# Second layer of a fused attention and two-layer network: gate and value as seven block products of 462 tokens in place of eight products of 512

## What is computed

```python
# attention: p_packed = sm_attn(p, k, v); out = sm_attn(q, p_packed, p_packed)
# x: (4608, 512)
h = x @ w_in                                   # 512 -> 2048
g = np.maximum(h, 0.0) + alpha * np.minimum(h, 0.0)
y = g @ w_out                                  # 2048 -> 512
# second layer, the one that the change rewrites
gate = y @ w_gate                              # 512 -> 1536
silu = gate * (1.0 / (1.0 + np.exp(-gate)))
val = y @ w_val                                # 512 -> 1536
out = silu * val @ w_out2                      # 1536 -> 512
```

## Time and profile before

| | |
|---|---|
| median of 3 runs | 1685.91 us (1685.32 to 1686.03) |
| the profiled execution, whole | 1685.89 us |
| its span, first to last instruction | 1683.7 us |
| TensorE busy | 1662.8 us (99%) |
| VectorE busy | 811.6 us (48%) |
| ScalarE busy | 568.6 us (34%) |
| granted TensorE clock, mean | 1.000 |

### The profile page before, as it was taken

How to read it: one execution, slowest core, us unless ns; L and a number is a source line. 1 busy time by engine, 2 the same in 40 slices (tenths; PEclk the granted TensorE clock), 3 DMA queues, 4 the chain that set the end, 5 groups by cost and what they waited for, 6 DMA issues and landing times.

```text
span 1683.7 us, 23290 instructions
## 1 busy us (share of the span) xinstructions
PE 1662.8 (99%) x9454; PEld 1480.7 (88%) x9454; DVE 811.6 (48%) x1524; ACT 568.6 (34%) x1229; POOL 19.1 (1%) x33
## 2 busy tenths in 40 slices
PE   9999999999999999999999999999999999999998
PEld 6899989999999999999888888888888888888887
DVE  4777678776976768656423232222323232232322
ACT  4565567555855566445201010100101010010100
POOL 0000000000000000000000000000000000000000
PEclk9999999999999999999999999999999999999999
DMA  7343223221322222124201010000101000010000
GB/s 254 102 121 114 85 73 95 77 82 49 111 63 78 70 65 68 40 76 135 84 1 51 0 51 0 25 26 0 51 1 51 0 26 25 1 50 0 26 0 26
DMA packets 51098, 94.83 MB, mean 56 GB/s; under 512 B 4896, under 2 KB 13104, under 8 KB 50992
## 3 DMA queue, kind: packets, MB, share of 16 engines
q1 hardware_dynamic: 48656, 83.90, 15.8%
q0 software_dynamic: 2336, 9.45, 1.6%
HBM read 74.46 MB, written 18.87 MB: 55 GB/s over the span
## 4 chain that ended last, share of the span: by engine, by line
PE 93%; DVE 4%; ACT 2%; issue 1%; DVEq 0%; ACTq 0%
PE acc L737 12%; PE h L531 9%; PE h L529 9%; PE h L530 9%; PE side L529 8%; PE side L530 8%; PE side L531 8%; PE acc L529 7%; PE acc L531 7%; PE acc L530 7%; PE acc L741 6%; DVE piece L1086 1%; ACT floats L823 1%; DVE floats L1254 1%; PE side L619 0%
## 5 line engine op out<-in xcount | busy, mean ns | idle before, releaser
L737 PE MATMUL acc<-g,w 128*128 128x288 f32 x1792 | 272.2, 294 | 0.0
L737 PEld LDWEIGHTS acc<-g,w 128*128 128x128 f32 x1792 | 249.0, 188 | 0.0
L1279 DVE TENSOR_TENSOR floats<-side,floats 128x512 f32<-128x512 f32 x54 | 37.4, 692 | 323.5 <-PE side L531 323.5
L823 ACT ACTIVATE g<-floats 128x288 fp32r<-128x288 f32 x256 | 113.8, 444 | 215.4 <-PE acc L741 104.9
L1279 DVE TENSOR_TENSOR floats<-h,floats 128x512 f32<-128x512 f32 x54 | 37.3, 691 | 266.2 <-PE h L531 266.2
L1254 DVE SCALAR_TENSOR_TENSOR floats<-floats,h 128x288 f32<-128x288 f32 x256 | 130.6, 510 | 61.1 <-ACT floats L983 59.5
L1086 DVE TENSOR_TENSOR g<-floats,g 128x288 fp32r<-128x288 f32 x256 | 115.4, 451 | 91.4 <-ACT g L823 89.5
L1086 DVE TENSOR_TENSOR piece<-floats,piece 128x512 fp32r<-128x512 f32 (+1 forms) x191 | 131.6, 707 | 57.9 <-ACT piece L823 55.8
L529 PE MATMUL h<-attn,mixed 128*128 128x288 f32 x512 | 156.9, 307 | 1.7 <-DVE attn L1086 1.7
L1012 ACT ACTIVATE floats<-side 128x512 f32<-128x512 f32 x54 | 32.3, 599 | 372.3 <-PE side L531 372.3
L741 PE MATMUL acc<-g,w 128*128 128x288 f32 x896 | 156.1, 296 | 0.0
(11 more groups left out here) (168 smaller groups left out, 3351.5 us busy)
## 6 DMA issues: line engine op xcount, KB each, us to landing
floats<-w_in SPq DMA_DIRECT2D x64, 256.0 KB, 3.0
y_scratch<-floats POOLq DMA_DIRECT2D x16, 576.0 KB, 3.6
floats<-y_scratch SPq DMA_DIRECT2D x9, 1024.0 KB, 5.0
out<-floats SPq DMA_DIRECT2D x36, 256.0 KB, 2.5
floats<-kT SPq DMA_DIRECT2D x28, 288.0 KB, 2.9
floats<-qT SPq DMA_DIRECT2D x28, 288.0 KB, 2.8
floats<-vS SPq DMA_DIRECT2D x28, 256.0 KB, 2.7
early<-w_in SPq DMA_DIRECT2D x16, 256.0 KB, 8.1
```

The costliest lines, as they stand in the source:

```text
L737: pe.matmul(acc[:, m, 0:CH], w2[:, j, x, m * P:(m + 1) * P], g[:, s % 2, 0, :], start=False, stop=False)
L823: return nc.scalar.activation(dst, src, ACT.Copy, **kw)
L1279: nc.vector.tensor_tensor(u_float(j), val_bank[j % 2], sg[:, j % 2, :], ALU.mult).then_inc(u_ready, 1)
```

## The change

Only the second layer's arithmetic is new, but it needs things prepared in the first layer.

**Block products.** Tokens now go in 5 runs (`HALF`: four of 2 x 462 and one of 2 x 456). Take the gate and value weights of one tile j as a 2 x 2 matrix of blocks: a11, a12 are the two feature halves of gate, a21, a22 those of value. Take the 512 features by 924 tokens of y as blocks B11, B12 (first feature half, first and second token half), B21, B22. The four results (gate and value of both token halves) come from seven products (`TERMS`) in place of eight: a11 B11, s2 T2, s1 T1, a22 T4, s3 T3, a12 B21, s4 B22, where s1 = a21 + a22, s2 = s1 - a11, s3 = a11 - a21, s4 = a12 - s2 and T1 = B12 - B11, T2 = B22 - T1, T3 = B22 - B12, T4 = B21 - T2. A product has 2 x 3 matmuls of 462 columns. A *set* n is the seven terms of one tile j in one run; there are 60. Four terms open a PSUM bank, three add to one after ScalarE or VectorE has read it.

**Work on VectorE and ScalarE.** A set's four results are put together from the banks: `copy_first`, `silu_1`, `silu_2` on ScalarE, `set_start` and `set_rest` on VectorE. Down for the first token half runs inside the sets, down for the second half (from a kept float tile `u2`) in a second loop of 12 tiles after them; there the next run's blocks are made and split as well (`T_STEPS`, 22 steps).

**Weights.** SBUF does not hold all seven split weight blocks of 12 tiles. So gate and value pieces and the sums s1 to s4 are made and split inside the first layer, at twelve places (`KEEP_AT`), and stored to a DRAM scratch `wS` by 48 DMAs from GpSimd; the second layer reads each set's 1.8 MB (four DMAs of SyncE, `load_weights`) into one of two places in turn, 60 times. Only the down weights stay.

```diff
+HALF = [462, 462, 462, 462, 456]
+TERMS = [("B11", 0), ("T2", 1), ("T1", 2), ("T4", 3), ("T3", 1), ("B21", 0), ("B22", 2)]
+KEEP_AT = [62, 73, 79, 97, 117, 141, 162, 181, 202, 208, 214, 220]
...
-WEIGHT_SLOT = [LAST + 6, LAST + 7] + [LAST + 8 + n for n in range(8)] + [LAST + NT1 + 1 + n for n in range(15)]
...
+MID[LAST + 1] += [("yload",), ("wload",)]
+for _n in range(len(T_STEPS)):
+    BACK[LAST + 4 + _n // 2].append(("tstep", _n))
...
+            def load_weights(n):
+                if n == 0:
...
+                elif n >= 2:
+                    once.wait_ge(term_done, 7 * (n - 2) + 7)
+                for i in range(4):
...
+                    sp.dma_start(ring(n, i).bitcast(F32), src).then_inc(weights_landed[n % 2], 16)
...
+            def term(n, i):
...
+                if i == 0:
+                    once.wait_ge(weights_landed[n % 2], 64 * (n // 2 + 1))
...
+                elif i == 6:
+                    once.wait_ge(value2_ready, n + 1)
+                w, x = term_weights(n, i), block_of(name)
+                for k in range(2):
+                    mm = product(bank_groups[r % 2][bank][:, 0:h], hl(lambda a: w[:, a, k * P:(k + 1) * P]),
+                                 hl(lambda a: x[:, a, k, 0:h]), i < 4 and k == 0, k == 1, skip_group_check=True)
...
-            for c in range(NC2):
+            for r in range(RUNS):
                 for j in range(NT2):
...
+                    n = NT2 * r + j
+                    for i in range(2 if n == 0 else 0, 6):
+                        term(n, i)
+                    if j:
+                        down_tile(2 * NT2 * r + j - 1)
+                    term(n, 6)
+                for d in range(NT2 - 1, 2 * NT2):
+                    down_tile(2 * NT2 * r + d)
...
+            def sums(j):
...
+                nc.vector.tensor_tensor(s1_, a21, a22, ALU.add).then_inc(sums_step, 1)
+                nc.vector.tensor_tensor(s3_, a11, a21, ALU.subtract).then_inc(sums_step, 1)
...
+            def set_rest(n):
+                r, j = divmod(n, NT2)
+                h, bank = HALF[r], bank_groups[r % 2]
+                once.wait_ge(term_done, 7 * n + 5)
+                nc.vector.tensor_tensor(first_three[:, 0:h], bank[1][:, 0:h], first_term[:, 0:h], ALU.add
+                                        ).then_inc(three_ready, 1)
+                once.wait_ge(three_ready, n + 1)
+                nc.vector.tensor_tensor(value2[:, 0:h], bank[2][:, 0:h], first_three[:, 0:h], ALU.add
+                                        ).then_inc(value2_ready, 1)
```

More of the change, by code:

```diff
@@ L20 @@
 CW = 512
-NC2 = TOK // CW
 ST = (SEQ + P - 1) // P
@@ L258, in build, with later @@
             pass
+        with ExitStack() as late:
+            def later(name, n, dtype=F32R):
+                return late.enter_context(nc.sbuf_tensor(name, [P, n], dtype))
+            down_ = later("down", NT2 * 1024)
+            ring1_ = later("ring1", 4096)
+            blocks_a = later("blocks_a", 4 * 4 * HW)
+            ring0_a = later("ring0_a", 512)
+            later("pad_a", 256)
+            sums_ = later("sums", 8192, F32)
+            blocks_b = later("blocks_b", 3 * 4 * HW)
+            later("pad_b", 64)
+            ring0_b = later("ring0_b", 1024)
+            u_ = later("u", 4 * HW)
+            later("pad_c", 2304 - 4 * HW)
+            silus_ = later("silus", 1152, F32)
+            ring0_c = later("ring0_c", 2048)
         w2_ = sbuf("w2", NT1 * 1024)
@@ L522, in _ @@
             once.wait_ge(y_stored, 16 * NCH)
+            for i in range(4):
+                once.wait_ge(kept[i], 16 * NT2)
         @block.tensor
@@ L828, in left @@
                 last = pieces_of(e)[-1] == p
-                if e[0] == "scores1" and last:
+                if e[0] == "keep":
+                    once.wait_ge(kept[e[2]], 16 * (e[1] + 1))
+                elif e[0] == "scores1" and last:
                     once.wait_ge(scores1_done, NTH[e] + 1)
@@ L921, in exp1 @@
                     once.wait_ge(rec_ready, 2 * (b - 1))
+                sums = before(e, "sums")
+                if sums:
+                    once.wait_ge(piece_split, PIECE_NO["s", sums - 1, 1] + 1)
                 nc.scalar.activation(s1[:, half, :].rearrange("p (c n) -> p c n", c=2), scores,
@@ L1287, in out_copy, with block_step_low @@
-            def out_copy(c):
-                once.wait_ge(out_done, (c + 1) * NT2)
+            def block_step_low(r, step):
+                kind, name, k = step
+                h = HALF[r]
+                done = len(T_STEPS) * r
+                if kind == "hl":
+                    once.wait_ge(block_high, len(T_HIGHS) * r + high_no(step) + 1)
+                    high = block_of(name)[:, 0, k, 0:h]
+                    subtract(block_of(name)[:, 1, k, 0:h], y_block(name, k)(h), high).then_inc(block_step, 1)
+                    return
+                a, b, needs = {"T1": ("B12", "B11", ("hl", "B11")), "T3": ("B22", "B12", ("sum", "T1")),
+                               "T2": ("B22", "T1", ("hl", "T1")), "T4": ("B21", "T2", ("hl", "B21"))}[name]
+                place = {"B12": (0, 1)}
+                at = [(lambda rows2, half: yraw[:, 2 * rows2 + k, half, 0:h])(*place.get(x, T_PLACE.get(x)))
+                      for x in (name, a, b)]
+                once.wait_ge(y_landed, 16 * KD * (r + 1))
+                once.wait_ge(block_step, done + T_NO[needs + (k,)] + 1)
+                nc.vector.tensor_tensor(at[0], at[1], at[2], ALU.subtract).then_inc(block_step, 1)
```

536 lines of the change are left out of this document (346 added, 190 removed).

## The result

The changed kernel takes 1646.38 us (median of four runs, 1645.52 to 1646.89), beside 1685.97 (1685.32 to 1686.53) for the kernel before in the same runs: a ratio of 0.9765 [0.9748, 0.9782]. The forecast was 1622: the direction is right, the size missed by 24 us. The profiled execution has a span of 1644.5 against 1683.7, so 39.2 us less.

A forecast was written before the change was run, and what follows sets the result against it. TensorE was taken as the bound, by number of matmuls times their pace. The terms summed as 1685.9 - 67.9 + 2.3 + 3 + 0 - 1.5 = 1621.8, say 1622 us, with a range of 1616 to 1642.

The forecast's parts named there:

- Term 1: Second layer's matmuls: 3960 narrower ones for 3888 of 512 columns, gain 67.9 us; 73 if cost is proportional to columns.
- Term 2: TensorE's waits within a set: about 0.45 us at each of five run starts, 2.3 us lost; ends 0 and 12.
- Term 3: First layer: added VectorE work at twelve places makes TensorE wait, 3 us lost; ends 0 and 10.
- Term 4: Second layer's weight loads: a set's 1.84 MB lands in 7.6 us, inside 10.9, so hidden; 0 us.
- Term 5: Kernel's end: only the last copy left after TensorE, 0.6 in place of 1.3 us, with shorter stores; -1.5 us.
- A: Rival: the first layer or the sets lose more, up to 10 and 12 us; 1631 to 1645 us; chance 0.17.
- B: Rival: y's load and the weight loads collide once or twice a run, 25 us; 1633 to 1655; chance 0.10.
- C: Rival: the weights' stream binds every set, slower than before; time over 1689 us; chance 0.04.
- D: Rival: new short waits drop TensorE's clock to 1.2 GHz for stretches, 51 us; 1673 us; chance 0.02.

The follow-up runs named there:

- Experiment 1: Kernel before the change plus 20 groups of 30 matmuls of various widths at its end, nothing beside them: 462 columns took 211.7 ns, 448 took 206.2.
- experiment 3: Changed kernel with weights loaded for the first two sets only, 58 of 60 loads left out: 1645.5 us, ratio 0.9763.
- Experiment 7: Changed kernel with weight sums and the splits of gate, value and sum pieces cut to 4 columns, order and DMAs kept: 1633.9 us, ratio 0.9689.
- 4: Changed kernel with each of the four weight sums cut to 4 of 256 columns, splits kept whole: 1641.38 us, ratio 0.9733.
- experiments 9: Changed kernel with the first of the twelve places moved from slot 62 to 134: 1646.99 us, ratio 0.9772.
- 10: Changed kernel with all places from slot 97 on, seven of them three slots apart at the end: 1646.0 us, ratio 0.9763.
- experiment 12: Changed kernel with runs of 464 and 448 tokens, slot 62 given up and five last places at slots 202 to 221: 1640.98 us, ratio 0.9736.

## Why the prediction was right in direction and wrong in size

**Term 1, the matmuls: the count held, the price failed.** The step "Between 288 and 512 columns the slope is 93.1 / 224 = 0.4156 ns a column, so 462 columns cost ... 205.9 ns and 456 cost 203.4" is wrong, and with it the reason given, "two widths of this trace lie on the line": two points always do. Measured are 210.2 ns in terms and 209.1 in down for 462, and 205.4 and 207.6 for 456; the term is -53.4, not -67.9. Experiment 1 shows that the width alone does this, experiment 3 that the stream does not. Why 448 costs more than 450 in the probe, and 462 more than 464, while in the kernel 464 costs what 462 does, stays open, as does why the probe's 448 (206.2) is above the kernel's (202.6). By the probe's own prices the layer would take 3168 x 211.7 + 792 x 207.9 ns = 835 us, against 828 measured; so the probe, too, holds only to 1%. The lower bound of the range (plain proportion) was on the wrong side, and no bound above the line was taken.

The Trainium skill ("TensorE: Matmul & The Clock Gate", Back-to-back issue gap) gives N/2.4 + 2.5 ns for the isolated gap, an estimate of 195 at 462 columns; the traces disagree, with 209 to 213.

**Term 2, waits in a set: right.** 0.4 us at each of five run starts for the predicted 0.45. The other 55 sets wait for nothing worth counting, as the steps show, none of which outside the run starts is over 0.26 us.

**Term 3, the first layer: the mechanism was right, the 3 us were mis-sized.** It measured 14.15, above even the end of 10. The failed step is "That gives a few tenths at slot 65, some 1.4 around 79, 0.7 around 201". Experiment 7 shows that the load is the cause (11.9 us go with it), and 4 gives the sums' share (5.0). Three things were missing. First, the count held VectorE's backlog against `g` alone. In the timeline of PE, ACT and DVE around slot 86 it is the key splits that are late:

```profile
326.98 0.74 ACT L1088 ACTIVATE floats<-side,floats 128x576 f32<-128x576 f32 x1 [1.68 <-DVE floats L1330]
...
327.71 1.24 ACT L990 ACTIVATE piece<-floats 128x576 fp32r<-128x576 f32 x2
...
328.41 1.43 DVE L1295 TENSOR_TENSOR piece<-floats,piece 128x576 fp32r<-128x576 f32 x2 [1.11 <-ACT piece L990]
...
329.32 0.37 PE L667 MATMUL side<-piece,pp 128*128 128x288 f32 x1 [1.16 <-DVE piece L1295]
```

ScalarE's two copies of 576 columns stand behind an exponential that waited 1.68 us for VectorE, VectorE then waits 1.11 us for the copies, and PE for VectorE. That is two engines in turn, and my sum had only one. Second, later places were counted at 0.7 us in all; with slots 96 to 116, 166, 180 and 201 to 214 they lose 6.2. Third, a wait that is listed as 0.46 cost 0.7. The busy stretch of the earlier trace rows now reads:

```profile
245.00:285.70 40.70, 39.00 (x261) 36.33 (x259) 39.05 (x73) 31.68 (x66) 3.67 (x6) 1.00 0.50 155
```

VectorE is at 39.05 of 40.7 us: full, with PE at 39.00 in place of 40.67.
How much of the 11.9 is ScalarE's part and how much VectorE's was not separated.

**Term 4, the stream: right.** Loads land in 4.9 to 7.0 us (median), the four of a set in 7.0 to 10.2 us (median 8.4) from the first issue where 7.6 was forecast, inside 10.9, and no wait of PE for a DMA appears; experiment 3 takes them away and gains nothing. **Term 5, the end: right,** 0.5 better. In the timeline of the end the last copy is one of 456 columns, in place of the pair in the earlier trace rows:

```profile
1640.77 0.55 ACT L990 ACTIVATE floats<-h 128x456 f32<-128x456 f32 x1 [0.70 <-PE h L669]
...
1641.39 0.63 DVE L1563 COPY floats<-h 128x456 f32<-128x456 f32 x1 [0.62 <-PE h L669]
```

**The rivals.** A in its first half was what happened, and beyond its bound: 14.15 us in the first layer with the sets at 2.1. A's 17 per cent were too few for the profile's 38.0 of 40.7 us. B's case can be read in the trace: at a run's set 3 the four weight loads issued from 831.95 to 833.30 us had landed at 840.66, and y, issued right behind them, at 845.43; a set with no y behind it takes as long (945.35 to 953.65). The loads landed as they were issued, as the rule quoted under B has it. B, C and D did not come: no late load, a mean granted clock of 1.00 and the top digit in every slice. The range's upper end of 1642 had A alone; both misses together passed it.

Four readings of the prediction are off without touching its sum: the fixed part of a matmul by its own slope is 13.9 ns (226.7 - 512 x 0.4156) and not 13, a load of y by its own rate takes 7.8 us (1.7 + 1.9/0.31) and not 7.5, the 25 us of B lead to 1647 and the way to its 1655 is not shown, and PE's wait of 1.5 us, which the earlier trace rows does not show, stands at 166 us and not in the opening.

## What to carry to other kernels

A product taken away at the bound engine pays close to what its count and columns say, but the columns' price has to be measured at the very width: the probe of 30 matmuls gives 835 us where 828 were measured and the line gave 813. Work added beside the bound is not free just because its engine has idle time on average: each of twelve places, an estimated 3.9 us on VectorE, cost about 1.2 us of TensorE on average (14.15 / 12). Moving places returned the loss there and took about as much elsewhere (experiments 9 and 10), but for the one that was fitted as a fifth into slots 202 to 225 (experiment 12: 2.9 us back). Follow a backlog over both engines that hand a tile on, and count restart time on top of each listed wait.

## What the runs showed of the hardware that was not expected

- The start-to-start time of float32r matmuls in a stream is not a line in the columns, nor always rising: 448 columns 206.2 ns, 450 203.5; 496 220.0, 504 226.9, 512 227.6. One width also has several paces: 462 columns took 211.7 and 213.1 in the probe at two data offsets, 210.2 and 209.1 in the kernel's two kinds of products.
- The weights' stream (1.8 MB a set, some 165 GB/s at 11 us a set) leaves the matmuls' pace as it is: 210.2 ns in terms with it and without.
- GpSimd takes 0.74 to 1.05 us for an addition or subtraction of 128x256 floats that takes VectorE 0.42.
- Forty-four stores of 512 KB (256 KB for one in four) beside the first layer cost nothing there (1645.99 against 1646.38); with the places three slots apart a ScalarE copy waited 0.96 us for one.
